# A scanned attention layer before a mixing layer: the check of the decay factors finishes one pair earlier, and the work between the two stages stands in another order

## What is computed

```
# attention, per batch, head and token t
state = alpha[t][:, None] * state + outer(k[t], v[t])
y[t]  = q[t] @ state
# mixing, x = y of all heads side by side: (4, 768, 384)
theta = x @ w_theta
y = einsum('ts,bsd->btd', w_tok_r, x * cos(theta)) + einsum('ts,bsd->btd', w_tok_i, x * sin(theta))
u = x + y
x = u + relu(u @ w_ch)
# gated convolution
h = relu(x @ w_in);  c = conv of 3 taps over the tokens of h
out = (h * sigmoid(c)) @ w_out
```

## Time and profile before

| what | us |
|---|---|
| median of three runs | 551.05 |
| lowest and highest run | 551.05, 551.81 |
| profiled execution, its own time | 551.51 |
| its span | 549.8 |
| TensorE busy in the span | 528.5 |
| VectorE, ScalarE, GpSimd busy | 447.3, 281.6, 71.9 |

### The profile page before, as it was taken

The page is one execution under the profiler, slowest core; times in us unless marked ns, Lnnn a source line. Parts: engine busy times, 40 slices in busy tenths (PEclk is TensorE's granted clock), DMA queues, the critical chain, the costliest instruction groups (busy, mean ns, idle before and its releaser), DMA issues.

```text
span 549.8 us, 11673 instructions
## 1 busy us (share of the span) xinstructions
PE 528.5 (96%) x4102; PEld 520.0 (95%) x4102; DVE 447.3 (81%) x792; ACT 281.6 (51%) x609; POOL 71.9 (13%) x70
## 2 busy tenths in 40 slices
PE   4999995999999999999999999999999999999997
PEld 3889895899999999999999999999999999999997
DVE  6899997488888666966596778799898988888884
ACT  4577777665553343444344463456454555546353
POOL 7567777300000000000000000000000000000000
PEclk9999999999999999999999999999999999999999
DMA  8899999352412102200107001302020202111011
GB/s 204 228 274 266 270 273 299 93 175 84 136 48 100 30 19 64 90 27 29 67 26 247 16 1 55 119 1 87 1 87 0 86 0 86 46 40 43 2 43 44
DMA packets 33946, 52.28 MB, mean 95 GB/s; under 512 B 3536, under 2 KB 23760, under 8 KB 33904
## 3 DMA queue, kind: packets, MB, share of 16 engines
q1 hardware_dynamic: 31168, 47.39, 29.0%
q10 hardware_dynamic: 2736, 4.33, 2.4%
HBM read 37.55 MB, written 14.16 MB: 94 GB/s over the span
## 4 chain that ended last, share of the span: by engine, by line
PE 91%; DVE 2%; DMA 2%; issue 2%; ACT 2%; POOL 1%; SPq 0%; DVEq 0%; POOLq 0%; ACTq 0%
PE y_bank L1306 27%; PE y_bank L1365 18%; PE x_bank L1352 9%; PE theta_bank L1352 9%; PE theta_bank L1293 7%; PE y_bank L1336 7%; PE weighed L1235 4%; PE x_sum L1212 3%; PE x_sum L1199 3%; PE turned L1221 2%; PE x_bank L1281 1%; DMA x_scratch<-x_rows 1%; DMA a_in<-in_a_first 1%; PE turned L1240 1%; DVE before L1006 1%
## 5 line engine op out<-in xcount | busy, mean ns | idle before, releaser
L1365 PE MATMUL y_bank<-first_w,z 128*128 128x384 f32 x576 | 109.9, 336 | 0.2 <-DVE z L1170 0.2
L1365 PEld LDWEIGHTS y_bank<-first_w,z 128*128 128x128 f32 x576 | 100.9, 188 | 0.5 <-DVE z L1170 0.5
L1306 PE MATMUL y_bank<-first_w,z 128*128 128x384 f32 x432 | 77.8, 338 | 0.0
L1306 PE MATMUL y_bank<-rest_w,z 128*128 128x384 f32 x432 | 76.8, 337 | 0.0
L1306 PEld LDWEIGHTS y_bank<-rest_w,z 128*128 128x128 f32 x432 | 74.5, 188 | 0.1
L1306 PEld LDWEIGHTS y_bank<-first_w,z 128*128 128x128 f32 x432 | 74.3, 188 | 0.0
L1150 DVE TENSOR_SCALAR x_rows<-out_rows,taps 128x384 f32<-128x384 f32 x64 | 26.8, 419 | 20.8 <-ACT out_rows L948 20.5
L948 ACT ACTIVATE out_rows<-theta_bank 128x386 f32<-128x386 f32 x32 | 15.8, 492 | 53.0 <-PE theta_bank L1352 53.0
L1293 PE MATMUL theta_bank<-theta_w,x_t 128*128 128x384 f32 x216 | 41.6, 337 | 1.2 <-DVE x_t L1043 1.2
L1235 PE MATMUL weighed<-q_scaled,k_scaled 64*128 64x128 f32 x384 | 35.0, 311 | 6.8 <-issue 3.8
L1153 DVE SCALAR_TENSOR_TENSOR x_rows<-out_rows,taps,x_rows 128x384 f32<-128x384 f32 x64 | 39.6, 619 | 2.3
(11 more groups left out here) (122 smaller groups left out, 957.8 us busy)
## 6 DMA issues: line engine op xcount, KB each, us to landing
k_in<-in_k_rows SPq DMA_DIRECT2D x32, 144.0 KB, 4.4
v_in<-in_v_tokens SPq DMA_DIRECT2D x16, 288.0 KB, 5.1
x_scratch<-x_rows SPq DMA_DIRECT2D x32, 144.0 KB, 4.0
x_in<-x_scratch SPq DMA_DIRECT2D x24, 192.0 KB, 2.6
a_in<-in_a_rows SPq DMA_DIRECT2D x30, 146.2 KB, 4.4
q_in<-in_q_rows SPq DMA_DIRECT2D x28, 144.0 KB, 4.5
y<-x_all SPq DMA_DIRECT2D x7, 576.0 KB, 3.2
u_scratch<-u_sum ACTq DMA_DIRECT2D x6, 576.0 KB, 3.4
```

Source lines behind the costliest of these rows:

```text
L1306: ins = pe.matmul(y_bank[2 * d + half][:, 0:HALF], z[s % 2][part][zp][:, d * P:(d + 1) * P], mixing_w(part, wp, s)[:, half_tokens(half)], ...
L1365: ins = pe.matmul(out_bank[half][t][:, 0:MODEL], g[k % 4][gp][:, t * P:(t + 1) * P], out_w[wp][f], start=f == 0 and i == 0, stop=f == FF_T ...
```

## The change

The verdict is made in the step of pair 14 in place of that of pair 15 (JUDGED_AT). The branch of PE and VectorE stays in the step of pair 15; SyncE's moves to that of pair 14. The sums of comparisons run ahead of the pairs: two of them stand in step 1 and two in step 7, so that pair 15 is compared and its values capped in step 13, and they stand ahead of the copies of x (`bring`, `keep`) and not behind them. Pair 14 has the cap of the chunk products, as before. `judge` stands behind `added`, in front of `scan_state`; PE no longer waits for a state there. Theta's weights are loaded in step 12, the pieces 0 and 1 in steps 13 and 14, the pieces 2 and 3 in the tail. `theta_high` and `theta_low` stand in step 15, and the low part is made by GpSimd; GpSimd no longer makes low parts of pieces. The high and low parts of the pieces 0 and 1 are made in the tail, the low parts by VectorE. The table load is now `waves`, behind `hold` of the first tile. The first tiles of x are loaded behind the verdict, as before, so one step earlier, and `store` of pairs 12 to 15 takes its batch from `x_batch`.

```diff
--- before.py
+++ after.py
@@ -64,7 +64,7 @@
 
 
 LEAST, MOST, LARGEST = 0.625, 1.375, 1e5
-JUDGED_AT = PAIRS - 1
+JUDGED_AT = PAIRS - 2
 
 LAG = 4
 HALF_TILES = HALF // P
@@ -211,7 +211,7 @@
 
 
 PLACES = """refill_piece refill_theta score scan_after scale_k spread cap by_token inside scan_before scale_q mask mask_late select added
-scan_state high bring keep low theta_high theta_low compare refill judge divert decide store halve hold turn theta angle sines
+scan_state high bring keep low theta_high theta_low compare waves refill judge divert decide store halve hold turn theta angle sines
 product round_z fill load load_first load_weight spare prepare mix sums end send join front gate split back_ff fetch""".split()
 Work = namedtuple("Work", PLACES, defaults=[nothing] * len(PLACES))
 
@@ -224,23 +224,18 @@
 
     def compared_in(i):
 
-        return [n for n in range(PAIRS) if n - (n >= JUDGED_AT - 1) == i]
+        return [n for n in range(PAIRS) if n - (n > 1) - (n > 8) == i]
 
     def pair_step(i):
         p, o = i - 1, i - 2
-        if i == JUDGED_AT:
-            for n in range(SPLIT_EARLY, LOADED_EARLY):
-                do.refill_piece(n)
         do.scan_after(i)
-        if i == JUDGED_AT:
-            do.judge()
         do.scale_k(i)
         do.spread(i)
-        if i < JUDGED_AT:
+        if i <= JUDGED_AT:
             do.cap(i)
         do.scan_before(i)
         do.scale_q(i)
-        if i == JUDGED_AT:
+        if p == JUDGED_AT:
             do.divert()
         if p >= 0:
             do.score(p)
@@ -253,24 +248,25 @@
             do.mask_late(p)
             do.select(p)
             do.added(p)
+            if i == JUDGED_AT:
+                do.judge()
             do.scan_state(p)
+        for n in compared_in(i):
+            do.compare(n)
+        if i == JUDGED_AT - 1:
+            do.cap(LAST_PAIR)
+        if i == LAST_PAIR:
+            do.theta_high()
+            do.theta_low()
         if o >= 0:
             for half in range(2):
                 do.bring(o, half)
                 do.keep(o, half)
-        for n in compared_in(i):
-            do.compare(n)
-        if i == JUDGED_AT - 1:
-            do.cap(LAST_PAIR)
         do.refill(i)
-        if i in (JUDGED_AT - 3, JUDGED_AT - 2):
-            do.refill_piece(i - (JUDGED_AT - 3))
-        if i == JUDGED_AT - 1:
+        if i == LAST_PAIR - 3:
             do.refill_theta()
-        if i in (JUDGED_AT - 2, JUDGED_AT - 1):
-            do.high(i - (JUDGED_AT - 2))
-        if i in (JUDGED_AT - 1, JUDGED_AT):
-            do.low(i - (JUDGED_AT - 1))
+        if i in (LAST_PAIR - 2, LAST_PAIR - 1):
+            do.refill_piece(i - (LAST_PAIR - 2))
         if i == JUDGED_AT:
             do.decide()
             do.load_first()
@@ -279,10 +275,11 @@
 
     def pair_tail():
         p, o = PAIRS - 1, PAIRS - 2
+        for n in range(SPLIT_EARLY, LOADED_EARLY):
+            do.refill_piece(n)
+        do.halve(0, 0)
+        do.high(0)
         do.score(p)
-        do.theta_high()
-        do.halve(0, 0)
-        do.theta_low()
         do.by_token(p)
         do.turn(0, 0)
         do.inside(o, 0)
@@ -290,9 +287,11 @@
         do.mask(p)
         do.mask_late(p)
         do.select(p)
+        do.low(0)
         do.hold(0, 0)
+        do.waves()
         do.theta(0, 0)
-        do.high(SPLIT_EARLY)
+        do.high(1)
         do.halve(0, 1)
         for half in range(2):
             do.bring(o, half)
@@ -302,6 +301,7 @@
         do.angle(0, 0)
         do.scan_state(p)
         do.sines(0, 0)
+        do.low(1)
         do.inside(p, 0)
         do.inside(p, 1)
         do.turn(0, 1)
@@ -312,6 +312,7 @@
         do.bring(p, 1)
         do.round_z(0, 0)
         do.keep(p, 1)
+        do.high(SPLIT_EARLY)
         do.theta(0, 1)
         do.store(p)
 
@@ -664,8 +665,7 @@
         def store(o):
             x_copied.done(sp, 2 * o + 1)
             b, first_head = o // PAIRS_PER_BATCH, 2 * (o % PAIRS_PER_BATCH)
-            if to_batch:
-                assert b == LAST
+            assert not to_batch or b == LAST
             for g in range(2):
                 at = (first_head + g) * HEAD_DIM
                 sp.dma_start(x_scratch[to_batch[0] if to_batch else b, at:at + HEAD_DIM, :], x_rows[o % 2][head(g), :]
@@ -781,9 +781,9 @@
             pool.affine_select(out=late, in_=late, compare_op=ALU.is_ge, fill=0.0, base=0,
                                pattern=[[0, len(BLOCKS_OF) - EARLY], [1, CHUNK]], channel_multiplier=-1).then_inc(selected.sem, 1)
 
-        def low(n):
-            piece_high.done(pool, n)
-            pool.tensor_tensor(pieces[n].low, raw_of(n), pieces[n].high.bitcast(F32), ALU.subtract).then_inc(piece_low.sem, 1)
+        def theta_low():
+            pool.wait_ge(theta_high_done, 1)
+            pool.tensor_tensor(theta_piece.low, theta_raw, theta_piece.high.bitcast(F32), ALU.subtract).then_inc(theta_low_done, 1)
 
         def load_weight(s):
             if s == 0:
@@ -812,7 +812,7 @@
         pool.memset(least[:, :], LEAST).then_inc(const, 1)
         pool.memset(most[:, :], -MOST).then_inc(const, 1)
         pool.memset(quarter[:, :], PI / 2).then_inc(const, 1)
-        program(pool, Work(scale_q=scale_q, scale_k=scale_k, select=select, low=low, load_weight=load_weight, prepare=prepare))
+        program(pool, Work(scale_q=scale_q, scale_k=scale_k, select=select, theta_low=theta_low, load_weight=load_weight, prepare=prepare))
 
     @block.scalar
     def _(act):
@@ -862,8 +862,8 @@
 
         def cap(n):
 
-            capped.done(act, n - 1)
-            if n < JUDGED_AT:
+            capped.done(act, n - 1 if n < JUDGED_AT else 2 * JUDGED_AT - n)
+            if n <= JUDGED_AT:
                 act.activation(excess[:, :], chunk_starts(after[n % 2][:, :], slice(0, CHUNKS), 1), ACT.Relu, bias=most[:, 0:1],
                                scale=MOST / LARGEST, accum_out=sums[:, PAIRS + n:PAIRS + n + 1]).then_inc(capped.sem, 1)
             else:
@@ -871,7 +871,7 @@
                 act.activation(shortfall[:, :, :], packed(a_in[n % 4][:, :], 1), ACT.Relu, bias=most[:, 0:1],
                                accum_out=sums[:, PAIRS + n:PAIRS + n + 1]).then_inc(capped.sem, 1)
 
-        def decide():
+        def waves():
             act.activation(unused[:, :], ident[:, 0:1], ACT.Sin)
 
         def halve(b, s):
@@ -982,7 +982,7 @@
         act.sem_inc(c_high.sem, MODEL_TILES)
         act.wait_ge(const, N_CONST)
         act.wait_ge(dve_const, N_DVE_CONST)
-        program(act, Work(by_token=by_token, mask_late=mask_late, keep=keep, spread=spread, cap=cap, high=high, theta_high=theta_high, compare=compare, decide=decide,
+        program(act, Work(by_token=by_token, mask_late=mask_late, keep=keep, spread=spread, cap=cap, high=high, theta_high=theta_high, compare=compare, waves=waves,
                           halve=halve, hold=hold, sines=sines, round_z=round_z, load_weight=load_weight, spare=spare,
                           prepare=prepare, sums=sums_of, send=send, fetch=fetch, front=front, gate=gating, split=split, back_ff=back_ff))
 
@@ -1081,10 +1081,6 @@
                 u_done.before(dve, b, 1)
             dve.tensor_copy(x_all[:, :, s * P:(s + 1) * P], x_in[s % 3][:, :, :]).then_inc(x_kept.sem, 1)
 
-        def theta_low():
-            dve.wait_ge(theta_high_done, 1)
-            dve.tensor_tensor(theta_piece.low, theta_raw, theta_piece.high.bitcast(F32), ALU.subtract).then_inc(theta_low_done, 1)
-
         def low(n):
             piece_high.done(dve, n)
             dve.tensor_tensor(pieces[n].low, raw_of(n), pieces[n].high.bitcast(F32), ALU.subtract).then_inc(piece_low.sem, 1)
@@ -1179,7 +1175,7 @@
         dve.memset(x_sum[:, :, :], 0.0).then_inc(dve_const, 1)
         dve.wait_ge(dve_const, N_DVE_CONST)
         program(dve, Work(scan_after=scan_after, scan_before=scan_before, judge=judge, mask=mask, scan_state=scan_state,
-                          divert=divert, theta_low=theta_low, turn=turn, angle=angles, fill=fill, product=product, round_z=round_z, load_weight=load_weight, sums=sums_of, end=end, spare=spare,
+                          divert=divert, turn=turn, angle=angles, fill=fill, product=product, low=low, round_z=round_z, load_weight=load_weight, sums=sums_of, end=end, spare=spare,
                           prepare=prepare, fetch=fetch, front=front, gate=gating, split=split))
 
     @block.tensor
@@ -1225,7 +1221,6 @@
         def judge():
             measured.done(pe, PAIRS - 1)
             capped.done(pe, PAIRS - 1)
-            stated.done(pe, JUDGED_AT - 2)
             pe.matmul(shortfalls, ones[:, :], sums[:, :], start=True, stop=True).then_inc(all_measured, 1)
 
         def score(p):
```

## The result

| | runs | median us | lowest to highest us | profiled execution, us | its span, us |
|---|---|---|---|---|---|
| before | 4 | 551.43 | 551.05 to 552.53 | 551.51 | 549.8 |
| after | 4 | 545.68 | 543.94 to 547.34 | 545.87 | 544.2 |

The ratio is 0.9892, with a 95% interval of 0.9857 to 0.9927. The gain is 5.8 us by the medians and 6.0 us by the ratio; 7.4 us were predicted for T0, and 543.6 us for the time. The runs after lie over 3.4 us, those before over 1.5 us. That width turned out to be the first clue.

The account below looks back on a forecast made before the run. PE's waits and low clock ahead of theta's first product were taken to bound the kernel; T0 7.4 us earlier takes 551.5 to 544.1 us, less 0.46 us for the median: 543.6 us, range 542.7 to 545.7 us.

Parts of the forecast that it names:

- T0: Start of theta's first product on PE, from which all work is a packed stream; predicted from 106.51 to 99.1 us.
- the terms: Up to pair 15's scores, 6.2 us: waits of 5.32 us plus the clock's 1.5 us, less 0.8 us of remaining wait.
- Comparisons: On ScalarE, ahead of the copies of x: they cost nothing, and the keys' wait of 1.10 us in step 14 goes.
- the slower rival: Comparisons wait for loads of a in steps 8 to 13; landing 7 us after issue cancels the gain; chance 0.03.
- The verdict and the branch: Verdict's sum on PE in step 14 without wait, 0.34 us on VectorE; pair 14's scores allowed from 89.7 or 90.2 us.
- q of pair 14: Its load stands behind theta's larger one in SyncE's queue: 0.7 us later, so GpSimd's product starts at 88.2 us.
- no wait over 1 us on PE: Sign of being right: after step 13, PE shows no such wait.
- The clock: PE's clock stays high, gaining 1.5 us; the rival that it still falls gives 545.1 us, chance 0.08.
- q later by half to one: Rival: pair 14's q, 0.5 to 1 us late, moves PE's chain: 544.1 to 544.6 us; chance 0.2, shared with GpSimd's gate.
- The place on GpSimd: Theta's low part on GpSimd in step 15 ends at 98.15 us, or 98.8 us beside VectorE, before PE is ready.
- factor of 1.23: Stretch of GpSimd's operation beside VectorE's subtractions, from selects of 0.64 and 0.79 us: theta's low part takes 3.3 us.
- The tail: Low parts of pieces 0 and 1 on VectorE, 0.91 us each, cost nothing; cover left before the mixing 0.2 us.

Follow-up runs that it names:

- e3: The kernel after with only the verdict in step 14 and the comparisons ahead; pieces, theta's work and sine table as in the kernel before: 546.13 us, ratio 0.9903.
- e4: The reverse: verdict, comparisons and cap as in the kernel before; loads, theta's work, pieces and sine table as in the kernel after: 550.20 us, ratio 0.9960.
- e12: e9 with the comparisons and the cap of pair 15 back behind the copies of x, still up to two steps ahead: 544.30 us, ratio 0.9862.
- e5: The kernel after with piece 0 loaded in step 12, piece 1 in step 13 and theta's weights in step 14: 545.20 us, ratio 0.9867.
- e6: The kernel after with theta's weights loaded in step 14, and pieces 0 and 1 in step 14 behind load_first and the store: 547.90 us, ratio 0.9919.
- e9: The kernel after with piece 0 loaded in step 13, theta's weights in step 14, piece 1 behind the store of step 14: 544.30 us, ratio 0.9853.
- e10: e9 with theta's low part moved from GpSimd back to VectorE, at the same place in step 15: 545.59 us, ratio 0.9880.
- e11: e9 with the sine table loaded at the end of step 15 on ScalarE, as before the change: 545.26 us, ratio 0.9871.
- e8: The kernel after, repeated unchanged beside e5 to e7: 547.09 us, ratio 0.9897.
- e1: The kernel after, run again unchanged: 547.01 us, ratio 0.9885.
- e7: e6 but with theta's weights loaded in step 13: 546.13 us, ratio 0.9897.
- e2: The kernel after without the fallback for decay factors out of range, its flag load and its jump: 546.69 us, ratio 0.9883.

## Why the prediction was right, and where it was off

**How near the number is.** The mechanism was forecast, but that the median lies in the range is in part luck: 545.68 us is 0.02 us below its end. Of the 16 runs of this kernel ten lie above 545.7 us, and its repetitions have medians of 547.01 and 547.09 us, against runs of the kernel before that were 0.9 and 0.4 us slower than here. Measured by ratios, which take such shifts out, the three (0.9892, 0.9885, 0.9897) lie inside the range's end (545.7 of 551.05 us, 0.9903) and all above the forecast (0.9865): the gain was overestimated by 1.1 to 1.7 us. Two slips in the sum are too small to matter: 88.2 + 1.79 is 89.99 us and not 89.95, and the terms add up to 6.0 us where the difference is 6.2, so 0.2 us of it has no term.

**What bounds the kernel, and the sign.** Right. From T0 on nothing changed: the mixing is 8.72 us behind it in both, and the kernel ends 5.6 us of span earlier for 6.0 us of T0. The 0.4 us between is behind the mixing's start and was not followed; in the kernels with a mixing 8.7 us behind T0 the way from T0 to the end varies from 443.3 to 443.7 us.

**Comparisons.** They cost nothing, as predicted, though loads of a did hold ScalarE up: by 0.35 us in step 13 and 0.78 us in step 12, 6.1 us in six waits of the whole trace, of which the longest took 1.6 us. One sign of being wrong (ScalarE waiting for loads of a in steps 8 to 12) thus came, and cost nothing: the scores of pair 13 start at 83.65 us, before at 83.68. The mechanism of the slower rival is there, below the point from which it decides. What I claimed for the edit was too much: most of the 1.10 us of the keys' wait came from the rounding of a piece. The wait stays with the comparisons moved alone (1.48 us, e3) and falls to 0.39 us with the pieces moved and the comparisons left (e4; 0.38 us in e12, where it is hidden), so the comparisons' share was at most 0.4 us.

**The verdict and the branch.** Right to 0.1 us: PE's sum at 87.55, VectorE's three operations ahead of the state's scan, the jump done by 89.6 us.

**q of pair 14: the term that was mis-sized.** "197 thousand bytes more at 280 GB/s are 0.7 us" gave 88.2 us. Measured were 88.42, 89.24 and 90.22 us in three executions of the same kernel, 0.9 to 2.7 us later than before. The step counted only the bytes added, from one row of before. The 1.15 us that PE waited for it also missed the sign "no wait over 1 us on PE". Theta's load itself took 6.8, 7.7 and 9.0 us to land in these three, and q of pair 14, behind it in SyncE's queue, up to 7.1, 7.8 and 8.9 us. But behind a piece it took not only the 6.2 us of the earlier trace rows: 6.9 and 7.4 us in e3 and e5. So the term left out is the scatter from execution to execution, of up to 2 us, and how much of the excess is theta's size is not shown. The DMA engines were nearly full (a share of 0.92 to 1.08 in the windows of 80 to 95 us); that a load which loses time there takes the next with it fits the numbers, and was not tested by itself. Up to a product of q at 87.9 us (the 89.7 of the branch less 1.79) the branch hides a late q; beyond that it goes whole onto PE.

**The clock.** I gave it 0.08 as a case of its own. It is not one of its own: it comes with a long wait of PE, which here a late q makes (and in e6 the late keys, 2.59 us). PE waits of 1.15 us and less ahead of the scores of pair 14 left the clock at 1.00 in the next window, in eight kernels; of 1.89, 2.00, 2.64 and 2.71 us brought it to 0.66 to 0.76 (e4, with 1.78 us behind the verdict's 2.67, to 0.56). The price was right: from the scores of pair 14 to those of pair 15 PE took 6.65 to 6.78 us in these four, and 5.22 to 5.24 us in e9 to e12. So the rival "q later by half to one" should have been "q later by one to two, and 1.5 us more for the clock": 546.1 to 547.1 us. Of the 16 runs of the kernel after in three measurements, seven lie at 543.9 to 545.9 us and nine at 546.8 to 548.9 us. The three profiled ones fit: 545.87 us with a clock of 1.00, 547.76 and 546.85 us with the low one. For the other thirteen no trace exists, so that they divide by q's landing is an inference; that executions also reach pair 13 at different moments (above) is a rival to it which no run excludes.

**The stop of 0.88 us.** In the execution profiled, T0 is 1.41 us later than predicted: 0.24 us by the scores of pair 14 and 1.26 us between them and the scores of pair 15, which the stop takes (behind them it is 0.06 us less than summed). It is no part of the kernel, since two other traces of it show none; what stops an engine there (PE for 0.88, GpSimd for 2.11 us in e5) stays open, and was not tried. Such stops of PE, at products of the same kind in step 10, are also in e5 (0.96 us), e6 (0.41 us) and e10 (1.24 us), all near 67.8 us, and these three are the ones that start pair 13 the latest (84.00 to 84.04 us).

**Theta.** The place on GpSimd held: 2.64 us from 95.99 to 98.63 us, inside the bounds of 98.15 and 98.8 us, and PE did not wait for it. My factor of 1.23 for the neighbour was wrong in size and in direction (below). The 1.20 us of theta's wait for VectorE, which the forecast gave to this edit, goes by another part of it: in e10 the low part is on VectorE, in step 15, and theta does not wait at all. So it was the place in the order that took the wait away, not the engine. The table's place is worth 1.0 us by e11, which I had left in that same wait.

**The tail.** Low(0) stretched to 1.33 us and low(1) of 0.93 us cost PE nothing; the low parts of z start at 108.09 us, 1.1 us ahead of the mixing.

## What to carry to other kernels

A large load was paid for here by the small ones behind it in the same queue. When you move one, look for the next transfer on which an engine already waits, and place the large one so that none stands behind it in a step that the critical path crosses (e9 gained some 2 us by this alone, by the medians). Two rivals that share a cause are not to be given chances apart: a wait of PE of 1.9 us and more and the clock's fall behind it came together every time. Where the runs of a kernel lie wider than those of its neighbours, one profile is not enough; take two or three before a cause is named.

## What the runs showed of the hardware

**VectorE and GpSimd shut each other out for a whole operation.** In the trace after, GpSimd's low part of theta (two operands from SBUF) ends at 98.63 us and VectorE's low part of x (two operands from SBUF) whose record starts at 97.74 us, ends at 99.05 us. This distance of 0.42 us, close to the operation's own length, returned, 0.41 to 0.42 us, in all nine traces where the two met, whatever the recorded length of x's low part: from 0.63 us (e8) over 1.17 and 1.93 us (e1, e9) to 2.75 us (e7). Alone it took 0.55 us (e10). GpSimd's operation was not stretched, 2.62 to 2.65 us in all. The other way round, GpSimd's select took 1.20 to 1.41 us where it began behind VectorE's low(0) with 0.7 us or more of that still to run (e1, e2, e4, e8, e10, e11), and ended 0.49 us behind it in all six; it takes 0.64 us otherwise. Where the select began first (after, e5), low(0) was the longer one, 1.33 and 1.07 us, and ended 0.81 us behind it. Even the row from which the factor of 1.23 came is such a meeting. VectorE's row beside the select of 0.79 us, before:

```profile
105.91 0.55 DVE L1043 TENSOR_TENSOR x_t<-x_in,x_t 128x384 fp32r<-128x384 f32 x1
```

It ends at 106.46 us, and the select ends at 106.95 us, again 0.49 us behind: a partial overlap of one lockout, and no ratio. VectorE's scans, whose second input lies in PSUM, ran beside GpSimd's products without such a lengthening: the scan at 83.38 us, 0.17 us of it beside one, took 1.75 us, and the one at 89.20 us, 0.9 us of it beside one, 1.74 us. This agrees with the Trainium skill (SBUF — State Buffer, section "SBUF: two separate sides"): the port pair that the two engines share is an exclusive lock; whoever starts first, a GpSimd operation or one of VectorE with two inputs in SBUF, holds it for the whole instruction, and the other blocks. I had turned a whole exclusion into a factor.

**The table load shows no tail here.** The operation behind the sine's table began 1.29 us after the table load did, with a load of 1.28 us. The Trainium skill (ScalarE: Activation LUTs, section "What ACT_TABLE_LOAD costs") gives about 1.28 us for the load, as here, and adds a drain of about 1.38 us. The trace shows none behind it, nor ahead: the copy before it ends at 100.30 us and the load starts at 100.32 us.
